# The start of a convolution and MLP kernel: halo rows by every fourth partition, both copies of w_in's last rows early, a first tile on six banks, low products put off, and a third tile transposed by TensorE

## The reference

```
w = softmax(weight_gen)                        # over the 7 taps; weight_gen [4, 4096, 8, 7]
x_pad = 6 zero rows ahead of x                 # x [4, 4096, 192]
c[s] = sum over k of w[s, head, k] * x_pad[s + k]
h = c @ w_in                                   # [16384, 192] @ [192, 2048]
out = maximum(0.01 * h, h) @ w_out             # [2048, 192]
```

## Time and profile before

| | |
|---|---|
| time, 3 runs | median 1063.36 us (1063.01 to 1063.74) |
| profiled execution | 1063.15 us, span 1061.3 us |
| granted TensorE clock, mean | 0.998 |
| TensorE busy | 1052.1 us, 99% |
| VectorE busy | 770.5 us, 73% |
| ACT busy | 632.5 us, 60% |
| GpSimd busy | 463.4 us, 44% |

### The profile page before, as it was taken

One profiled execution on the slowest core, in us unless ns is written; L12 is line 12 of the kernel. 1 busy time (PEld: TensorE's weight loads), 2 busy tenths in 40 slices (PEclk: granted clock), 3 DMA queues, 4 the chain that ended last, 5 costly groups with the idle time before them and its releaser, 6 DMA issues.

```text
span 1061.3 us, 20777 instructions
## 1 busy us (share of the span) xinstructions
PE 1052.1 (99%) x8787; PEld 720.8 (68%) x8787; DVE 770.5 (73%) x1109; ACT 632.5 (60%) x1332; POOL 463.4 (44%) x369
## 2 busy tenths in 40 slices
PE   8999999999999999999999999999999999999998
PEld 3666676676667667667766766766676676677666
DVE  7999867787775877758687677877758777586711
ACT  6766555565556556556655555655565565566554
POOL 0003444455445445435544444554454454455433
PEclk9999999999999999999999999999999999999999
DMA  8101303102121121212203031021321212111010
GB/s 259 48 30 34 94 19 94 33 24 86 33 79 34 39 76 28 79 34 65 63 16 93 19 94 33 23 87 33 79 33 34 82 29 79 33 34 33 16 33 16
DMA packets 67685, 57.03 MB, mean 54 GB/s; under 512 B 56524, under 2 KB 60748, under 8 KB 65608
## 3 DMA queue, kind: packets, MB, share of 16 engines
q1 hardware_dynamic: 67468, 55.41, 18.6%
q10 hardware_dynamic: 124, 0.29, 0.1%
HBM read 29.34 MB, written 12.58 MB: 40 GB/s over the span
## 4 chain that ended last, share of the span: by engine, by line
PE 95%; DVE 3%; SPq 1%; DMA 1%; ACT 0%; issue 0%; POOL 0%; DVEq 0%; ACTq 0%; POOLq 0%
PE out_ps L856 32%; PE out_ps L865 15%; PE h_ps L814 10%; PE h_ps L815 10%; PE h_ps L817 10%; PE h_ps L816 10%; PE h_ps L830 6%; DMA rawD<-in_moe_w_in_dram 1%; DVE gl L582 1%; DVE conv L540 1%; SPq L286 0%; DVE prod L533 0%; SPq L289 0%; DVE wo L562 0%; PE t_ps L856 0%; ACT wo_abs L353 0%
## 5 line engine op out<-in xcount | busy, mean ns | idle before, releaser
L255 POOL TENSOR_TENSOR gl<-g,gh 128x512 f16<-128x512 f32 x360 | 461.3, 1309 | 590.0 <-ACT g L382 590.0
L380 ACT ACTIVATE gh<-h_ps 128x512 f16<-128x512 f32 x512 | 319.1, 623 | 391.4 <-PE h_ps L833 391.4
L856 PEld LDWEIGHTS out_ps<-wo,gh 128*128 128x128 f16 x4064 | 329.0, 98 | 54.2 <-issue 53.4
L856 PE MATMUL out_ps<-wo,gh 128*128 128x192 f16 x4064 | 359.4, 246 | 0.3 <-DVE wo L562 0.3
L582 DVE TENSOR_TENSOR gl<-g,gh 128x512 f16<-128x512 f32 x152 | 132.8, 887 | 269.8 <-ACT g L382 269.8
L382 ACT ACTIVATE g<-h_ps 128x512 f32<-128x512 f32 x512 | 323.7, 632 | 0.0
L540 DVE TENSOR_TENSOR conv<-conv,prod 128x768 f32<-128x768 f32 x186 | 229.6, 1234 | 1.1
L533 DVE TENSOR_TENSOR prod<-xbuf,taps 128x768 f32<-128x768 f32 x186 | 202.7, 1102 | 0.0
L814 PE MATMUL h_ps<-xT,whA 128*128 128x512 f16 x504 | 191.5, 380 | 0.5 <-ACT g L382 0.5
L815 PE MATMUL h_ps<-xT,wlA 128*128 128x512 f16 x504 | 191.5, 380 | 0.0
L817 PE MATMUL h_ps<-xT,whA 128*128 128x512 f16 x504 | 191.5, 380 | 0.0
(11 more groups left out here) (82 smaller groups left out, 410.3 us busy)
## 6 DMA issues: line engine op xcount, KB each, us to landing
xbuf<-in_x_dram SPq DMA_DIRECT2D x15, 1344.0 KB, 5.9
out_dram<-stage SPq DMA_DIRECT2D x31, 384.0 KB, 2.3
taps<-in_weight_gen_dram SPq DMA_DIRECT2D x16, 224.0 KB, 5.9
xT_again<-xT SPq DMA_DIRECT2D x30, 64.0 KB, 2.1
rawO<-in_moe_w_out_dram SPq DMA_DIRECT2D x4, 384.0 KB, 9.9
rawA<-in_moe_w_in_dram SPq DMA_DIRECT2D x2, 512.0 KB, 8.5
xbuf<-in_x_dram SPq DMA_DIRECT2D x2, 384.0 KB, 6.9
rawD<-in_moe_w_in_dram SPq DMA_DIRECT2D x1, 512.0 KB, 7.4
```

Source lines behind the costliest of these rows:

```text
L255: nc.gpsimd.tensor_tensor(gl[:, f % RING, :], g[:, f % RING, :], gh[:, f % RING, :], ALU.subtract).then_inc(s_gl_p, 1)
L380: nc.scalar.activation(gh[:, f % RING, :], h_ps[f % GROUP][:], ACT.Prelu, scale=SHRINK, alpha=SLOPE).then_inc(s_gh, 1)
L856: nc.tensor.matmul(out_of(m, j), gh[:, f % RING, j * P:(j + 1) * P], wo[:, f, part, :], start=f == 0 and (j % 2 == 0 or alone) and part == ...
```

## The change

- **Halos.** `load_halos` takes a list of partition ranges with a step of 4: three DMAs of 32 partitions (1, 5, ... 125 and so on), then one for each batch with 7 partitions. SP issues the first four, ACT the last three.
- **Last rows of w_in.** The first copy stays on SP, the second goes as one DMA of 512 KB on ACT's queue, after ACT's two exponentials. SP no longer loads the second copy's two parts.
- **VectorE's start.** The softmax of tap half 1 beyond its first two operations stands behind the products of tile 0. In `first_tile` the low parts of A1 and D1 and the spread for w_out stand ahead of conv1's first operations.
- **ACT's start.** Three `abs_wo` instead of two stand ahead of `hi_of_x(0)`, the fourth ahead of the high parts of A1 and D1.
- **Six banks.** In tile 0 block f goes to bank f mod 6 of h_ps 0 to 3, t_ps and t2_ps; tile 1's first transpose waits for g of block 10.
- **xT_again** of the tiles that TensorE transposes is copied by GpSimd.
- **Low products.** Those of tile 0's third group (blocks 8 to 11) come after the high ones of its fourth. VectorE's first gl of tile 1 waits for them (s_late_lo), as does ACT's first gh of tile 1 for gl of block 8.
- **Third tile.** BY_PE is 3: tile 2 is transposed by TensorE too, with VectorE's `take_transposed(2)` among tile 3's convolution.

```diff
-        BY_PE = 2
+        BY_PE = 3
+        first_banks = [bank[:] for bank in h_ps] + [t32_ps[:], t2_32_ps[:]]
+        def h_of(m, f):
+            return first_banks[f % len(first_banks)] if m == 0 else h_ps[f % GROUP][:]
-            for first, last in ((1, 17), (17, 32)):
-                p0, p1 = b * PART_SEQ + first, b * PART_SEQ + last
-                queue.dma_start(xbuf[p0:p1, 0, 0:HALO * D], x_rows[p0 - 1:p1 - 1, (T_PART - HALO) * D:]
+        def load_last_rows(queue, half):
+            queue.dma_start(rawD[half * DR:(half + 1) * DR, :], w_in[P:D, :]).then_inc(s_rawD[half], DMA)
+        HALOS = [(c, P) for c in (1, 2, 3)] + [(b * PART_SEQ + 4, (b + 1) * PART_SEQ) for b in range(B)]
+        def load_halos(queue, halos):
+            for first, end in halos:
+                queue.dma_start(xbuf[first:end:4, 0, 0:HALO * D], x_rows[first - 1:end - 1:4, (T_PART - HALO) * D:]
...
+            for t in range(BY_PE):      # GpSimd
+                pool.wait_ge(s_xT_a, 2 * (t + 1))
+                nc.gpsimd.tensor_copy(xT_again[DR:P, t % 2, :].rearrange("p (j c) -> p j c", c=P), xT[0:DR, t % 2, :, 1, :]
+                                      ).then_inc(s_xT_p, 1)
...
-            load_last_rows(0, 0, FF, 0)      # SP
+            load_last_rows(sp, 0)
-            load_last_rows(1, 0, PIECE, 1)
-            load_last_rows(1, PIECE, FF, 2)
...
-                if b == 1:      # ACT, take_transposed
-                    nc.scalar.copy(xT_again[DR:P, t % 2, :], t_ps[0:DR, b, :]).then_inc(s_xT_a, 1)
+                    if n == NG:      # ACT, leaky
+                        act.wait_ge(s_gl_v, NF - RING + f + 1)
             exp_half(0)
             exp_half(1)
+            load_last_rows(act, 1)
...
-            for n in range(2):
+            for n in range(N_PIECES - 1):
                 abs_wo(n)
             hi_of_x(0)
             split_hi(PIECES[0])
             take_transposed(0, 0)
             split_hi(PIECES[1])
             take_transposed(0, 1)
+            abs_wo(N_PIECES - 1)
             for piece in PIECES[2:4]:
                 split_hi(piece)
-            for n in range(2, N_PIECES):
-                abs_wo(n)
...
                 take_transposed(0)      # VectorE, first_tile
+                lo_pieces(2, 4)
+                w_top(1)
                 conv1(0, 1)
-                lo_pieces(2, 4)
-                conv1(1, 2)
-                w_top(1)
-                conv1(2, 3)
                 w_scales(1)
+                conv1(1, 3)
...
+                dve.wait_ge(s_late_lo, 1)      # second_tile
                 group(NG)
...
-            for ops in (range(0, 2), range(2, N_SOFTMAX)):
-                for half in range(2):
-                    for n in ops:
-                        softmax0(half, n)
+            for half in range(2):
+                for n in range(2):
+                    softmax0(half, n)
+            for n in range(2, N_SOFTMAX):
+                softmax0(0, n)
...
             nc.vector.tensor_tensor(prods0[5], prods0[5], prods0[6], ALU.add).then_inc(s_prod0, 1)
+            for n in range(2, N_SOFTMAX):
+                softmax0(1, n)
...
-                    dst = h_ps[f % GROUP][:]      # TensorE, hidden
-                    if n > 0:
+                    dst = h_of(m, f)
+                    if m > 0:
                         pe.wait_ge(s_g, m * NF + f - GROUP + 1)
+                    elif f >= len(first_banks):
+                        pe.wait_ge(s_g, f - len(first_banks) + 1)
...
-                if n + 1 == NG:      # TensorE, step
-                    hidden_by_pe(1)
+                if i == NG - 1 and m + 1 < BY_PE:
+                    hidden_by_pe(m + 1)
...
-                project(n)
+                project_hi(n)
+                if i == NG - 2 and m + 1 < BY_PE:
+                    transpose_hi(m + 1)
+                if n == 2:
+                    return
+                if n == 3:
+                    project_lo(2)
+                if n < NG * TILES - 1:
+                    project_lo(n)
+                else:
+                    last_lo()
```

More of the change, by code:

```diff
@@ L133, in dynconv_mlp @@
         s_rawA = [sem(f"s_rawA{n}") for n in range(2)]
-        s_rawD = [sem(f"s_rawD{n}") for n in range(3)]
+        s_rawD = [sem(f"s_rawD{n}") for n in range(2)]
         s_rawO = [sem(f"s_rawO{n}") for n in range(4)]
@@ L272, in _ @@
             sp.wait_ge(s_halo_zero, 1)
-            for b in range(B // 2):
-                load_halos(sp, b)
-            def load_last_rows(half, first, last, n):
-                sp.dma_start(rawD[half * DR:(half + 1) * DR, first:last], w_in[P:D, first:last]).then_inc(s_rawD[n], DMA)
-            load_last_rows(0, 0, FF, 0)
+            load_halos(sp, HALOS[0:4])
+            load_last_rows(sp, 0)
             for half in range(2):
@@ L337, in split_hi @@
                 raw, hi, _ = pieces[piece]
-                if piece[0] == "D" and piece[1] < 2:
-                    act.wait_ge(s_rawD[piece[1] + 1], DMA)
+                if piece == ("D", 0):
+                    act.wait_ge(s_rawD[1], DMA)
                 act.wait_ge(s_w_scale, scales_done(piece))
@@ L436, in _ @@
             act.wait_ge(s_halo_zero, 1)
-            for b in range(B // 2, B):
-                load_halos(act, b)
+            load_halos(act, HALOS[4:])
             exp_half(0)
             exp_half(1)
+            load_last_rows(act, 1)
             act.wait_ge(s_w_sum, 2)
@@ L588, in step @@
                 last = m == TILES - 1
+                late = m == 2 and i < 2
+                if late:
+                    lo_of_g(n * GROUP + GROUP - 1, n % NG * GROUP + GROUP - 1)
                 if m % 2 == 0 and m + 2 < TILES:
@@ L609, in step @@
                         convolve(m + 2, sum(CONV_AHEAD_IN[b] for b in range(2, i)) + k)
-                elif n > 2 * NG:
+                elif not late:
                     lo_of_g(n * GROUP + GROUP - 1, n % NG * GROUP + GROUP - 1)
@@ L720, in second_tile @@
                 lo_of_x(2)
-                for n in range(6):
+                for n in range(2):
                     convolve(3, n)
+                take_transposed(2)
                 group(NG + 3)
-                for n in range(6, CONV_AHEAD):
+                for n in range(2, CONV_AHEAD):
                     convolve(3, n)
@@ L728, in _ @@
             dve.wait_ge(s_taps0, DMA)
-            for ops in (range(0, 2), range(2, N_SOFTMAX)):
-                for half in range(2):
-                    for n in ops:
-                        softmax0(half, n)
+            for half in range(2):
+                for n in range(2):
+                    softmax0(half, n)
+            for n in range(2, N_SOFTMAX):
+                softmax0(0, n)
             dve.wait_ge(s_softmax0[0], N_SOFTMAX)
-            dve.wait_ge(s_x0, (1 + 2 * B) * DMA)
+            dve.wait_ge(s_x0, (1 + len(HALOS)) * DMA)
             for k in range(K):
@@ L829, in last_rows @@
                     if f % 2 == 0:
-                        ins = nc.tensor.matmul(h_ps[f % GROUP][:], wlD[0:DR, c], xT[0:DR, par, :, 1, :],
+                        ins = nc.tensor.matmul(h_of(m, f), wlD[0:DR, c], xT[0:DR, par, :, 1, :],
                                                start=False, stop=True)
                     else:
-                        ins = nc.tensor.matmul(h_ps[f % GROUP][:], wlD[DR:P, c], xT_again[DR:P, par, :],
+                        ins = nc.tensor.matmul(h_of(m, f), wlD[DR:P, c], xT_again[DR:P, par, :],
                                                start=False, stop=True)
@@ L843, in wait_lo, with project_hi @@
                     pe.wait_ge(s_gl_p, ((m - EARLY) * NF + f) // GROUP * (GROUP - 1) + f % GROUP + 1)
-            def project(n):
+            def project_hi(n):
                 m, i = n // NG, n % NG
-                fs = range(i * GROUP, (i + 1) * GROUP)
-                for f in fs:
+                for f in range(i * GROUP, (i + 1) * GROUP):
                     pe.wait_ge(s_gh, m * NF + f + 1)
@@ L896, in step @@
                     wait_w_in(n + 1)
-                if n + 1 == NG:
-                    hidden_by_pe(1)
+                if i == NG - 1 and m + 1 < BY_PE:
+                    hidden_by_pe(m + 1)
                 elif n + 1 < NG * TILES:
```

72 lines of the change are left out of this document (37 added, 35 removed).

## The result

The changed kernel takes 1070.70 us (median of 6 runs, 1068.86 to 1071.34), the one before beside it 1063.27 (1063.01 to 1064.62): a ratio of 1.0065, 95% interval [1.0052, 1.0078]. It is slower by 7.4 us where 4.0 were forecast, and lies above the range's end of 1069.5. Its profiled execution took 1070.48 us, with a span of 1068.7.

What follows compares the result with a forecast made beforehand. VectorE's run from 26.25 to 53.84 us was taken to bound the start, TensorE the steady part. Start 2.1, low products 1.0 and third tile 0.9 sum to 4.0 us: 1067.15 profiled, 1067.4 beside the median; 8-in-10 range 1065.0 to 1069.5.

Steps and rivals of the forecast that it cites:

- First term: Start of tile 0: x_scale of tile 1, with the gl and ACT's g behind it, comes 2.1 us later.
- 0.8 us of delay: Landing of w_out's third piece: delay by the second copy, chosen between 0 and 2.1 us, putting hi_of_x(0) at 19.7.
- The upper bound from the slow rate: Start: with the second copy at 186 GB/s the piece is 2.1 us late and the start's loss 3.4 us.
- The rule of the Trainium skill cited there: Last rows' loads: two half-partition transfers serialize, only 6% faster together; delay 2.1 us, sum 1.3 us higher.
- contention and clock: Rival, chance 0.18: slow second copy holds up rawA and w_out, 1068.7 us; TensorE's half clock 0.9 us more, 1069.6.
- Halos, 0: VectorE's first products: earlier start only lengthens its wait for ACT's sums over w_in; worth 0.
- the 1.05 us of cover: VectorE's wait for ACT's sums over w_in, up to 15.88 us: hides as much as 1.05 us of halo delay.
- The clock step: TensorE may fall to 1.2 GHz while waiting over 2 us for hi_of_x: 1.7 us, 0.9 after ACT's lead.
- Six banks, 0: Tile 0's hidden products: 0.47 us and most of TensorE's hole go, but VectorE holds the chain; worth 0.
- Low products, +1.0: End of tile 0: 0.3 us gained before ACT's g is late, 1.32 us of products still to do; net +1.0.
- The wait that the edit adds on VectorE: VectorE's first gl of tile 1 waits for the put-off products: covered by about 2 us, cost 0.
- Third tile, +0.9: Tile 2's transposes by TensorE: +0.7 us and a wait of 0.2 us, between 0.7 and 1.2.

Runs made afterwards that it cites:

- a_rows_old: Changed kernel with only the loads of w_in's last rows as they were before: 1067.94 us, ratio 1.0047.
- a_loads: Changed kernel with both the halo loads and the loads of w_in's last rows as before: 1067.70 us, ratio 1.0041.
- a_halos_old: Changed kernel with only the halo loads as they were before: 1070.57 us, ratio 1.0064.
- a_third_late: Changed kernel with VectorE's copy of tile 2's transposed low values behind six convolution operations instead of two: 1068.50 us, ratio 1.0045.
- b_banks: Kernel before with only the first tile's hidden products in six banks: 1063.65 us, ratio 1.0003.
- b_third_late: Kernel before with the third tile transposed by TensorE, VectorE's copy behind six convolution operations instead of two: 1064.19 us, ratio 1.0008.
- b_rows: Kernel before with only the second copy of the last rows loaded whole on ACT's queue: 1065.14 us, ratio 1.0013.
- b_order: Kernel before with only the first tile's new order of abs_wo, softmax and conv1, loads as before: 1064.60 us, ratio 1.0014.
- b_putoff: Kernel before with only the low products of tile 0's third group put off: 1064.29 us, ratio 1.0012.
- b_third: Kernel before with only the third tile transposed by TensorE, VectorE's copy behind two convolution operations: 1066.31 us, ratio 1.0024.

## Why the prediction was wrong

The direction and the places were right: the start, the put-off products and the third tile, and no gain from six banks. Two of the three terms were mis-sized: the start, by the landings, and the third tile, by a wait on VectorE that was not followed.

- **First term, 2.1 us against 3.5.** Its chain is as described: three sums of w_out, hi_of_x(0) right behind them, VectorE's wait for A1 (1.11 us), TensorE's waits for VectorE's low pieces. From hi_of_x(0) to tile 1's it took 30.49 us, 0.10 more than before, where the steps gave 0.4 more; the scatter between traces is larger. The failed step is the landing of w_out's third piece: 0.8 us of delay were taken from between 0 and 2.1, and the third sum, which waited for it, began at 20.20, 2.3 us behind the old landing at 17.94. Pieces of w_out took 11.5 us to land where a_rows_old, with the old loads of the last rows, has 8.6, and hi_of_x(0) came 3.43 us late, not 1.7. Not only that piece was late: rawD's first copy was issued 1.07 us later, behind the slower halo issues (4.67 against 3.60), and took 8.3 us to land, not 7.4, and with it ScalarE's whole row of sums came 2.04 us later, where the forecast had left it in place. The upper bound from the slow rate was the one to take: from 10 to 14 us the loads passed at 211 and 215 GB/s. The rule of the Trainium skill cited there (page "SBUF — State Buffer", section "Can I just issue two DMAs to hit both halves?"), of two transfers to either half of the partitions that hardly run faster together than one, agrees with the rows: from 8 to 10 us the changed kernel, with both copies on their way, passed 213 GB/s, and a_rows_old, with one, 207, though both had other loads on their way as well. That was the first half of the rival "contention and clock", whose first term of 3.4 us is nearly what was measured.

```profile
8.00:10.00 2.00, 0.00 (x0) 0.00 (x0) 0.58 (x1) 0.00 (x0) 0.00 (x0) 1.00 0.93 213
8.00:10.00 2.00, 0.31 (x1) 0.30 (x2) 1.42 (x2) 0.00 (x0) 0.00 (x0) 1.00 0.91 207
```

- **Halos, 0.** a_rows_old against a_loads gives 0.2 us of medians, and a_halos_old 0.1. So 0 is right for the medians, but not for the reason given. The products began 1.75 us later than before (9.42 against 7.67), more than the 1.05 us of cover, and VectorE waited 1.43 us for sums at half clock; what hides them is that ScalarE waits for loads at the same time. In the profiled execution the halos' chain even ended last, 0.29 us behind the third sum over w_out, and in a_third_late's, with the same start, it ended last too (ScalarE waited 0.50 us for x_scale). The clock step that the rival "contention and clock" had, while TensorE waits for hi_of_x, is in none of the changed kernel's rows; its clock fell earlier, at 10 to 12 us, after it had waited for the halos. The rival's step is in a_halos_old's trace.
- **Six banks, 0.** Right in time (b_banks). The half clock at 28 us is off the path as the prediction has it: VectorE ran on without a wait beside it, b_third_late, with none there, has tile 1's hi_of_x at 48.46 against 48.39, and b_rows and b_order, with none either, the same 1012.9 in the steady column, so TensorE carries no loss from it past tile 1.
- **Low products, +1.0 against 1.2.** Right, with ACT as what is late next. The wait that the edit adds on VectorE cost nothing: in b_putoff VectorE is not idle before its first gl of tile 1.
- **Third tile, +0.9 against 2.5.** The 0.9 is right for what it counted: b_third_late measures it. The step that failed is one not made. The working followed TensorE and ScalarE and didn't ask what is queued behind VectorE's `take_transposed(2)`: four gl and seven convolution operations of tile 3. It stood there 4.54 us in the changed kernel. ScalarE passed the delay on, waiting for tile 4's and 5's softmax and for tile 3's scale:

```profile
107.14 0.58 ACT L360 ACTIVATE taps<-taps 128x448 f32<-128x448 f32 x1 [4.83 <-DVE taps L491]
...
115.68 1.49 ACT L381 ACTIVATE xs<-conv,x_scale 128x192 f16<-128x192 f32 x4 [4.06 <-DVE x_scale L531]
```

Behind each of them stand the gh and g that free TensorE's banks. That is 1.6 us, shown by the pairs b_third and b_third_late, and the changed kernel and a_third_late.

Sum: 3.5 + 1.2 + 2.5 = 7.2, and the span grew by 7.4. The 0.2 us over are not assigned; VectorE's moved gl in tile 2, which no run has alone, may be in them.

Shown by runs with one part alone or one part back are 2 to 3 us for the last rows' loads, 1.2 for the low products, and 0.9 and 1.6 for the third tile. Open is how the start's loss is shared between the pieces that land late and the halos' chain at half clock, since both end within 0.3 us of each other.

## What to carry to other kernels

When a wait is put into an engine's program, list what is queued behind it on that engine, even where the engine isn't the bound: 4.5 us of VectorE, a quarter idle, became 1.6 us of TensorE. In a start that is bound by loads, count every byte ahead of the piece that is waited for last, whichever queue it goes by, at the slowest rate seen, and look for the second chain that ends just behind the first: mending one alone may give nothing. And find a point behind which the time to the end is steady: span less that point splits a change into parts that one profile can weigh.
